# Decay work of a scan, attention and MoE kernel laid out over the three steps of a half batch

## The reference

```python
mag = np.sqrt(a_re * a_re + a_im * a_im)
scale = np.minimum(mag, 0.999) / (mag + 1e-06)
a_re_n, a_im_n = (a_re * scale, a_im * scale)
for t in range(S):                      # S = 768, per batch (4) and head (8), D = 48
    S_re, S_im = (a_re_n*S_re - a_im_n*S_im + kv, a_re_n*S_im + a_im_n*S_re)
    y[:, :, t] = np.einsum('bhd,bhde->bhe', q[:, :, t], S_re)
# x = y as 3072 x 384; top-1 MoE over 8 experts (384 -> 1024 -> 384, relu, gate);
# then ((x @ m1) * (x @ m2)) @ m3 @ m_out
```

## Time and the profile before

| | |
|---|---|
| median of 3 executions | 996.34 us (994.27 to 997.73) |
| the profiled execution | 999.18 us |
| its span | 997.4 us |
| attention's steps (first `weigh_inputs` of each) | from 36.73 to 316.73 us |
| folds and first item | 342.5 to 378 us |
| MoE and last products | 378 us to the end |

### The profile page before, as it was taken

The page is one execution under the profiler, slowest core; times in us unless marked ns, Lnnn a source line. Parts: engine busy times, 40 slices in busy tenths (PEclk is TensorE's granted clock), DMA queues, the critical chain, the costliest instruction groups (busy, mean ns, idle before and its releaser), DMA issues.

```text
span 997.4 us, 17948 instructions
## 1 busy us (share of the span) xinstructions
PE 919.1 (92%) x6799; PEld 813.5 (82%) x6799; DVE 446.1 (45%) x705; ACT 410.0 (41%) x618; POOL 398.3 (40%) x230
## 2 busy tenths in 40 slices
PE   2889989789898699999999999998999999999996
PEld 2579888788787567889999999997898989898986
DVE  4888899799785531432222222222313131313130
ACT  5879888778572322322223223221313131212121
POOL 6647755965854416647256627700010101010101
PEclk9999999999999899999999999999999999999999
DMA  9624452553282346343353444301010101000000
GB/s 240 135 54 84 81 105 59 127 104 67 72 272 100 101 163 233 116 164 104 104 167 105 124 154 155 125 25 48 0 65 0 64 1 64 1 32 1 32 1 32
DMA packets 160152, 91.82 MB, mean 92 GB/s; under 512 B 128576, under 2 KB 152896, under 8 KB 160064
## 3 DMA queue, kind: packets, MB, share of 16 engines
q1 hardware_dynamic: 147344, 67.81, 25.4%
q10 hardware_dynamic: 9648, 13.30, 4.1%
q0 software_dynamic: 3072, 9.49, 2.4%
HBM read 71.77 MB, written 18.81 MB: 91 GB/s over the span
## 4 chain that ended last, share of the span: by engine, by line
PE 70%; DVE 14%; POOL 6%; issue 5%; ACT 4%; another core or an unknown queue 1%; ACTq 0%; DVEq 0%; POOLq 0%
PE psum L1929 20%; PE psum L1888 13%; PE psum L1866 13%; PE psum L1941 10%; PE psum L425 6%; PE psum L1771 3%; DVE arena L1169 2%; DVE arena L1247 2%; PE psum L1706 1%; DVE arena L1198 1%; PE psum L1732 1%; POOL x_by_expert L715 1%; POOL arena L684 1%; DVE wfold_half L1581 1%; DVE arena L1177 1%
## 5 line engine op out<-in xcount | busy, mean ns | idle before, releaser
L1929 PE MATMUL psum<-x2t,ring 128*128 128x512 f32 x864 | 197.1, 389 | 0.0
L1929 PEld LDWEIGHTS psum<-x2t,ring 128*128 128x128 f32 x864 | 162.1, 188 | 33.4
L425 PE MATMUL psum<-arena 128*128 128x128 f32 x925 | 127.6, 279 | 31.4 <-DVE arena L1169 19.1
L818 POOL DMA_INDIRECT out_dram<-arena x24 | 23.1, 962 | 320.9 <-ACT arena L1147 317.4
L425 PEld LDWEIGHTS psum<-arena 128*128 128x128 f32 x925 | 107.5, 143 | 47.4 <-POOL arena L652 19.0
L1866 PE MATMUL psum<-ring,f_xt 128*128 x558 | 137.3, 400 | 4.4 <-DVE f_xt L1555 4.4
L1888 PE MATMUL psum<-ring,f_ht 128*128 x744 | 138.7, 341 | 2.0 <-DVE f_ht L1561 2.0
L1888 PEld LDWEIGHTS psum<-ring,f_ht 128*128 128x128 f32 x744 | 129.7, 190 | 2.4 <-issue 2.3
L1866 PEld LDWEIGHTS psum<-ring,f_xt 128*128 128x128 f32 x558 | 103.7, 190 | 26.0 <-issue 4.9
L1596 DVE TENSOR_TENSOR ab_f<-psum,a_sb 128x512 f32<-128x512 f32 x48 | 33.2, 692 | 204.6 <-ACT a_sb L1137 204.6
L1941 PE MATMUL psum<-wfold_half,ab 128*128 128x384 f32 x576 | 102.8, 336 | 0.0
(11 more groups left out here) (180 smaller groups left out, 1372.6 us busy)
## 6 DMA issues: line engine op xcount, KB each, us to landing
stage<-in_moe_w_dram SPq DMA_DIRECT2D x16, 1536.0 KB, 7.2
y_dense<-arena ACTq DMA_DIRECT2D x31, 194.0 KB, 3.1
arena<-x_by_expert ACTq DMA_DIRECT2D x28, 194.0 KB, 2.4
arena<-y_dense SPq DMA_DIRECT2D x24, 194.0 KB, 3.5
arena<-in_a_re_dram SPq DMA_DIRECT2D x24, 192.0 KB, 3.8
arena<-in_a_im_dram SPq DMA_DIRECT2D x24, 192.0 KB, 3.7
...
```

What stands on the lines that cost most here:

```text
L425: return nc.tensor.transpose(psum[:, bank, c0:c0 + P], src, ident)
L1929: last = mm(psum[:, bank + j % 2, :], m_half[m][x][:, kc, j * P:(j + 1) * P], x2t[y][:, kc, :], start=(kc == 0 and x + y == 0), stop=(kc = ...
```

## The change

Within a half batch the calls of the decay work stand in other steps: `unit_check` and `seed` in the first (i = 0), `clip`, `ratio`, `damp` and `ratio_check` in the second, `inverse`, `angle` and `sines` in the third; `sum_angles` stands behind `root_prod` in the first. The ratio has one tile for even and one for odd units (`s4`), and its check squares it in place. In the start the sines and cosines of unit 0 stand ahead of `seed(1)`, and the first two late `fold_t` and `fold_cols` stand ahead of the last routing. Steps 0 to 2 have an order of their own.

The diff, without the tiles' addresses:

```diff
@@ -164 +165 @@ def unit_cols(t):
+        s4 = [s4_even, cols(take(ND), ND)]
@@ -399 +400 @@ def ratio_of(m):
-            return (s3_second, s4_second) if m == 1 else (s3, s4)
+            return s3_second if m == 1 else s3, s4[m % 2]
@@ -403 +404 @@ def prepared(k):
-            return {0: [K], 1: [K + 1, K + 2]}.get(k, [k + AHEAD] if k + AHEAD < K * U else [])
+            return {0: [], 1: [K, K + 1], 2: [K + 2, K + 3]}.get(k, [k + AHEAD] if k + AHEAD < K * U else [])
@@ -731 +732 @@ def step(k):
-                if k == 0:
-                    root_prod(0, 0)
-                    ratio_seed(1)
-                    root_prod(0, 1)
-                    root_prod(0, 2)
-                elif i == 0 and n < U:
+                if i == 1 and k > 1 and p < U:
+                    ratio_seed(p)
+                if i == 0 and n < U:
@@ -738 +737 @@ def step(k):
+                if i == 0 and 0 < n < U - 1:
+                    sum_angles(n + 1)
@@ -743 +744 @@ def step(k):
+                    ratio_seed(1)
@@ -744 +746 @@ def step(k):
+                if k == 1:
+                    ratio_seed(2)
@@ -747 +749 @@ def step(k):
-                if i == 1 and p < U:
-                    ratio_seed(p)
-                if i == 2 and p < U:
-                    sum_angles(p)
@@ -838 +837 @@ def seed(m):
-                    act.wait_ge(r_checked, m)
+                    act.wait_ge(ratio_done, m)
@@ -904 +901 @@ def ratio_check(m):
-                act.wait_ge(ratio_done, m + 1)
-                t, ratio_m = ratio_of(m)
-                S.activation(t, ratio_m, ACT.Square).then_inc(sq_ratio, 1)
+                act.wait_ge(theta_done, m + 1)
+                t = ratio_of(m)[1]
+                S.activation(t, t, ACT.Square).then_inc(sq_ratio, 1)
@@ -968 +965 @@ def step(k):
-                if k and prepared(k - 1):
+                if k >= 2 and prepared(k - 1):
@@ -971 +969 @@ def step(k):
+                if k == 2:
+                    whole_turns(1, 2)
+                    seed_inv_log(1)
@@ -974 +973 @@ def step(k):
-                        sines(n)
@@ -977 +977 @@ def step(k):
+                    if k == 0:
+                        whole_turns(1, 0)
@@ -980 +981 @@ def step(k):
-                if i == 1 and p < U:
-                    seed(p)
-                    damp(p)
-                if i == 2:
+                    if 0 < n and p < U:
+                        seed(p)
+                if i == 1 and k > 1:
+                    if m < U:
+                        ratio_check(m)
+                    if p < U:
+                        damp(p)
+                if i == 2 and k > 2:
@@ -989 +993 @@ def step(k):
-                for a in prepared(k)[:-1]:
-                    whole_turns(*divmod(a, K))
@@ -999 +1002 @@ def step(k):
-                if i == 0:
-                    if m < U:
-                        ratio_check(m)
-                    if n < U:
-                        prod_end(n)
+                if k == 1:
+                    seed(2)
+                    ratio_check(1)
+                    damp(2)
+                if k == 2:
+                    seed_inv(1)
+                    trig()
+                    angle(2)
+                if i == 0 and n < U:
+                    prod_end(n)
@@ -1007 +1015 @@ def step(k):
-                    if m < U:
+                    if k > 1 and m < U:
@@ -1010 +1019 @@ def step(k):
+                    sines(m)
@@ -1013 +1021 @@ def step(k):
-            act.wait_ge(consts, 9)
@@ -1017 +1026 @@ def step(k):
+            act.wait_ge(consts, 9)
@@ -1019 +1027 @@ def step(k):
-            ratio_check(0)
@@ -1026 +1033 @@ def step(k):
-            seed(1)
-            damp(1)
-            fold_rows(0, fold_out)
@@ -1032 +1038 @@ def step(k):
+            fold_rows(0, fold_out)
+            logs()
+            seed(1)
+            damp(1)
+            trig()
+            ratio_check(0)
@@ -1037 +1049 @@ def step(k):
+            fold_cols(EARLY, m3t_late)
+            fold_cols(EARLY + 1, m3t_late)
@@ -1055 +1067 @@ def square_root(n):
-            fold_cols(EARLY, m3t_late)
@@ -1057 +1069 @@ def square_root(n):
-                if i + 1 < NJ:
+                if EARLY < i < NJ - 1:
@@ -1173 +1185 @@ def unit_check(m):
-                if m:
-                    dve.wait_ge(theta_done, m)
-                    dve.wait_ge(r_checked, m)
+                if m >= 2:
+                    dve.wait_ge(r_checked, m - 1)
@@ -1366 +1377 @@ def step(k):
-                    a = prepared(k - 1)[-1]
-                    turn(*divmod(a, K))
-                    if a % K == K - 1:
-                        ends(a // K)
+                    turn(*divmod(prepared(k - 1)[-1], K))
@@ -1372 +1379 @@ def step(k):
-                if i == 2 and p < U:
-                    ratio(p)
@@ -1377 +1384 @@ def step(k):
+                if k < K * U:
+                    weigh_inputs(n, i)
+                    turn_k(n, i)
@@ -1379 +1388 @@ def step(k):
-                    weigh_inputs(0, 0)
+                    unit_check(1)
@@ -1382 +1390 @@ def step(k):
-                    scan(1, 0)
-                    turn_k(0, 0)
@@ -1385 +1391 @@ def step(k):
-                elif k < K * U:
-                    weigh_inputs(n, i)
-                    turn_k(n, i)
@@ -1390 +1394 @@ def step(k):
-                if k:
-                    for a in prepared(k):
-                        scan(*divmod(a, K))
-                        if a != prepared(k)[-1]:
-                            turn(*divmod(a, K))
+                for a in prepared(k):
+                    scan(*divmod(a, K))
+                    if a % K == K - 1:
+                        ends(a // K)
+                    if a != prepared(k)[-1]:
+                        turn(*divmod(a, K))
+                    if a == K + 2:
+                        ratio(2)
@@ -1397 +1404 @@ def step(k):
-                if i == 1 and p < U:
+                if i == 0 and k and p < U:
@@ -1398 +1406 @@ def step(k):
+                if k == 1:
+                    unit_check(2)
+                if i == 1 and p < U:
@@ -1399 +1410 @@ def step(k):
+                    if k > 1:
+                        ratio(p)
@@ -1420 +1431 @@ def step(k):
-            unit_check(1)
@@ -1760 +1772 @@ def fold_t(i, m3s):
+                    if i == EARLY and half == 0:
+                        pe.wait_ge(att_masked, 2 * K * U)
@@ -1813 +1827 @@ def step(k):
+            fold_t(EARLY, m3_late)
+            fold_t(EARLY + 1, m3_late)
@@ -1836 +1851 @@ def step(k):
-            fold_t(EARLY, m3_late)
-            for i in range(EARLY, NJ):
-                if i + 1 < NJ:
+            for i in range(EARLY, NJ - 1):
+                if i > EARLY:
@@ -1840 +1854 @@ def step(k):
-                    fold(i, m3t_late, mo_late)
+                fold(i, m3t_late, mo_late)
```

More of the change, by code:

```diff
@@ L131, in bass_attention_moe_mlp @@
         n_at = top[0]
-        s1, s2, s3, s4 = [cols(take(ND), ND) for _ in range(4)]
+        s1, s2, s3, s4_even = [cols(take(ND), ND) for _ in range(4)]
         body_at = top[0]
@@ L146, in bass_attention_moe_mlp @@
         a_second = [cols(second_at + x * ND, ND) for x in range(2)]
-        s3_second, s4_second = [cols(second_at + (2 + x) * ND, ND) for x in range(2)]
-        assert second_at + 4 * ND <= top[0]
+        s3_second = cols(second_at + 2 * ND, ND)
+        assert second_at + 3 * ND <= top[0]
         half_way = top[0]
@@ L730, in step @@
                     scatter_rows((k - PICKED - 2) // C, 0, K)
-                if k == 0:
-                    root_prod(0, 0)
-                    ratio_seed(1)
-                    root_prod(0, 1)
-                    root_prod(0, 2)
-                elif i == 0 and n < U:
+                if i == 1 and k > 1 and p < U:
+                    ratio_seed(p)
+                if i == 0 and n < U:
                     for x in range(K):
                         root_prod(n, x)
+                if i == 0 and 0 < n < U - 1:
+                    sum_angles(n + 1)
                 if i == 0 and k >= PICKED + 3 and (k - PICKED - 3) % C == 0:
                     scatter_rows((k - PICKED - 3) // C, K, C)
-                if 0 <= k < K * U:
+                if k < K * U:
                     turn_q(n, i)
                 if k == 0:
+                    ratio_seed(1)
                     sum_angles(1)
+                if k == 1:
+                    ratio_seed(2)
                 if i == 0 and p < U:
                     add_squares(p)
-                if i == 1 and p < U:
-                    ratio_seed(p)
-                if i == 2 and p < U:
-                    sum_angles(p)
             add_squares(0)
@@ L862, in whole_turns @@
                 act.wait_ge(phase_done, k0 + 1)
-                if n == 1:
-                    act.wait_ge(r_checked, 2)
                 if n >= 2:
@@ L1377, in step @@
                     state(k - 2)
+                if k < K * U:
+                    weigh_inputs(n, i)
+                    turn_k(n, i)
                 if k == 0:
```

(21 more changed lines are left out.)

## The result

The changed kernel takes 1003.17 us in the median (1002.99 to 1004.17, 4 executions) beside 995.31 (993.50 to 997.73) for the kernel before: a ratio of 1.008, interval 1.0055 to 1.0104. It is 8 us slower; the forecast was 6.8 us faster, and 1003.17 lies outside both the range of 984 to 994 and that of 977 to 1001. The profiled execution took 1004.17 us with a span of 1002.5.

The account below looks back on a forecast made before the run. TensorE was taken to bound the kernel, VectorE its i = 1 steps. Steady steps -14.1, start +10.3 and tail -3.0 gave -6.8 us off the median of 996.34: 989.5, range 984 to 994, with rivals 977 to 1001.

Parts of the forecast that it names:

- the start: Steps 0 to 2, walked instruction by instruction: step 3 comes 8.7 us late, with 1.6 for the low clock +10.3 us.
- the steady steps: Steps 3 to 18: without `unit_check` and `clip`'s wait, i = 1 steps fall to TensorE's length; -14.1 us in all.
- the tail: Around the last routing: 16 transposes move into time TensorE waits, so the first fold starts 3.2 us earlier; -3.0 us.
- 1.6 us for one such stretch: Start, step 2: TensorE's lower clock after an idle stretch, counted once on the path, adds 1.6 us.
- it fits: i = 0 steps: VectorE, busy 5.65 of 8.68 us, has room for the added `unit_check` of 1.4 us.
- the two nearly cancel: Steps 12 and 18: longer wait for `turn_q` against `sum_angles` no longer colliding with `inverse`; 12 to 13 becomes 11.9 us.
- The walk: Steps 0 to 2 traced through the engines' queues: step 2 starts at 69.7 us, step 3 at 91.2 instead of 82.52.
- signs of being wrong: Step 3 starting before 86, L1181 still over 3 us, or `mask` waiting for `whole_turns` in i = 0.
- The rival in which the i = 1 steps keep their collisions: `ratio_seed` slips and meets `clip` again; steady gain only 7 us, total 996.6, no change; chance 0.15.
- so 12 to 14 gains 24.6 - 21.9 = 2.7: Steps 12 and 13: 12 to 13 becomes 11.9 us and 13 to 14 10.0, a gain of 2.7 us.
- so I let it bound nothing here: Steady steps: ScalarE has 10.0, 9.1 and 11.0 us in i = 0, 1, 2, under TensorE's 11.1, so never bounds.
- the slower rival: ScalarE's late copies hold TensorE: `sines` last in i = 2 delays `turn` and `mask`; +11 us, 1007; chance 0.14.

Follow-up runs that it names:

- e1: Changed kernel, but in step 2 ScalarE makes `seed_inv(1)`, the table and `angle(2)` ahead of the copies, as before: ratio 1.0015 to the kernel before.
- e2: Changed kernel plus 44 transposes on TensorE that nobody reads, in its wait of step 2: ratio 1.006 to the kernel before.
- e9: Changed kernel with `seed(2)`, `damp(2)`, `seed_inv(1)`, the table, `angle(2)` ahead of the start's copies and chunk 5's `decay_cols` ending TensorE's step 1: ratio 0.9988.
- the old start: Steps 0 to 2 on all engines as in the kernel before, from step 3 on the changed kernel with its tail: ratio 0.9936.
- e13: Changed kernel with the old start, plus unread transposes on TensorE ahead of `scores(12)`, `scores(18)` and the count: ratio 0.9937 to the kernel before.
- e14: Changed kernel with the old start, and GpSimd's `add_squares` waits for `unit_check` in steps 9 and 15: 987.5 us beside 999.15, ratio 0.9881.

## Why the prediction was wrong

The forecast for the time missed by 14.7 us. By parts it missed 5.8 in the start, 9.3 in the steady steps and 0.1 in the tail. Three of its steps failed: the low clock at 1.6 us "for one such stretch", where it took 5.0 in the start and 2.5 more in steps 12 and 18; the i = 0 steps, in which "it fits" was true of step 6 and not of 9 and 15; and "the two nearly cancel" for steps 12 and 18.

**The start, +10.3 forecast, +16.1 measured.** The mechanism stood in part: `seed_inv(1)` and `angle(2)` behind the copies cost 6.7 us (e1). The walk has step 2 at 21.5 us, 10.4 over before, and names these copies alone for it. But 7.5 us over before remain without them: `seed_inv_log(1)` waits for the scan of chunk 5, now in step 2, and the walk has that scan, "until 73.3", but not this wait. The mis-sized term is "1.6 us for one such stretch", the low clock. It came three times. On the path: `outputs(0)` 1.95 instead of 1.08; `outputs(1)` 1.95 and 2.55 instead of 1.08 and 1.95; then 2.07, 1.88 and 2.79 instead of 1.06, 1.04 and 2.06. That is 0.9 + 1.5 + 2.6 = 5.0 us, 3.4 more than I gave; e2 took the last part away and won 2.7. (The walk's own 1.8 us for `phases(2, 0)`, 84.1 to 85.9, is 0.7 over the 1.06 that it takes at the full clock, and no row gave that.) Another 2.1 are in step 0 (step 1 at 53.92, forecast 51.8); the experiments that share this step 0 have it between 52.05 and 53.82, so part of it is chance. The walk also gave "66.0" as the end of ScalarE's work in step 1 and never asked about `decay_cols` of chunk 5, on which `clip(2)` waits as well (e9: 3.7 us once ScalarE is out of the way). The remaining 4 to 5 us between e9 and the old start I haven't split by a run; in e9 step 2 is 7.5 us longer than before and step 0 2.9 shorter. None of the signs of being wrong came up, though step 3, to come near 91, came 7.6 us later.

**The steady steps, -14.1 forecast, -4.8 measured: the larger miss.** The collision that was to go went; what failed is what I gave for the i = 0 steps.
- "So step 4 to 5 falls from 13.7 to 11.1": it is 11.09, and `clip`'s second half takes 1.36 us. Steps 10 and 16 gain 3.5 each for 3.9. Steps 6 to 8 gain 2.1 for 1.3. The rival in which the i = 1 steps keep their collisions is refuted.
- "so 12 to 14 gains 24.6 - 21.9 = 2.7": it loses 0.8, and 18 to 19 loses 2.6 for 0.5. I had the wait for `turn_q` behind `sum_angles` and the scatters, and charged it against `inverse`: "the two nearly cancel". They don't: `turn_q` ends 2.1 and 1.7 us later in steps 12 and 18. What I left out altogether is that TensorE comes out of the wait slow: 1.7 us for `scores(12)`, 0.8 for `scores(18)`. e13 gives back 1.4 and 1.5 us. Together 5.6 us of the missing 9.3.
- "In the i = 0 steps `unit_check` is added to a VectorE that is busy 5.65 of 8.68 us, so it fits": true of step 6, not of 9 and 15. There `pick` already took 2.67 us in the kernel before, unseen, since nothing stood close behind it. With `unit_check` between it and `mask` VectorE is busy 12.19 of 12.47 us. It costs 1.2 us twice; e14 removes it and wins 1.7 twice. With what follows in steps 12 and 18, taking this one collision away shortens steps 3 to 19 by 8.3 us (e14).
- ScalarE: "so I let it bound nothing here". `whole_turns` behind `sines` holds VectorE's `turn` for 1.41 us in step 8, and steps 8 and 14 are 0.6 us longer each. This is the mechanism of the slower rival, ScalarE's late copies, at 1.1 us instead of its 18: that its 1007 is the time nearest to the measured one is luck.

**The tail, -3.0 forecast, -3.1 measured**, but for reasons half as told, so the number is in part luck. The fold starts 3.5 us sooner against the count and loses 2.0 of it to the low clock. The passage to the MoE gives 1.6 back, against "by a chain that doesn't move": the first rows are sent for 25.3 us behind the count, before 27.3.

The Trainium skill, "SBUF — State Buffer", section "Who interferes with whom", says that a VectorE instruction with two SBUF inputs and a GpSimd one that reads SBUF exclude each other, and that the order of issue, not the shape, decides who waits. The trace agrees: 48 elements waited out 2.65 us of GpSimd. I had used the rule for the collision that goes and only in a rival for the ones that come.
